# Gate segments, numerators and magnitudes reordered in the first iterations of an xLSTM-plus-MoE kernel

## The chip, the cores and the metric

The kernel runs on one core of one Trainium2 chip. The metric is the device time of one execution in microseconds (us), lower is better. The engines named below are PE (TensorE), DVE (VectorE), ACT (ScalarE), POOL (GpSimd) and SP (SyncE, which here only issues DMAs).

## The reference

Three parts follow each other on the same 1536 tokens (2 batches of 768), 320 wide (8 heads of 40):

```python
# 1: matrix-memory recurrence, per batch and head, over t
m_new = max(f_gate + m, i_gate)
f_stab, i_stab = exp(f_gate + m - m_new), exp(i_gate - m_new)
C = f_stab * C + i_stab * outer(v, k);  n = f_stab * n + i_stab * k
y = sigmoid(o_gate) * (C @ q) / max(|n . q|, 1)
# 2: rational activation between two matmuls, d_ff 2048
h = x @ w_in;  P = a0 + a1 h + a2 h^2 + a3 h^3;  Q = 1 + |b0||h| + |b1| h^2
x = (P / (Q + 1e-6)) @ w_out
# 3: RMS norm, gated unit, d_ff 1536
xn = x / rms(x) * rms_g;  y = (silu(xn @ w_gate) * (xn @ w_val)) @ w_out
```

## The kernel before, in words

Each engine has its own instruction list, written out by hand; the engines meet only at semaphores, and an engine that waits holds everything behind it in its list. There is no scheduler: the order in the code is the order on the engine.

The recurrence is computed in chunks of L = 128 steps. There are NT = 12 iterations `it`; iteration `it` is chunk c = it // 2 of batch b = it % 2. Per iteration PE makes the causal mask (`causal`, L1477) and adds the log weights (`log_weights`, L1492) in PSUM; ACT takes their exponential E (`weights`, L826); PE forms `scores` (L1467); DVE weighs the values (`weigh`, L1169) and multiplies scores by E (`probs`, L1176); PE forms the numerators within the chunk (`intra`, L1518), the part from earlier chunks (`carry`, L1505) and the state update (`updates`, L1528). DVE copies or adds up the numerators (`combine`, L1194/L1197), computes the reciprocal denominator (`denominators`: magnitude L1218, maximum with 1 L1219, reciprocal L1225) and writes the state (`state`, L1208/L1210). POOL multiplies by the output gate (`gated`, L576) and by the reciprocal (`normalised`, L585 and L588), decays the state (`decay`, L519) and fills a column of ones in each loaded value tile (`ones`, L509), for which `weigh` waits (semaphore `v_ready`). For the two last iterations ACT computes the magnitude instead of DVE (`magnitude`, L891).

The gates are [16, 768] and are handled in three segments, SEG: steps 0 to 127 (chunk 0, iterations 0 and 1), 128 to 255 (chunk 1, iterations 2 and 3), and the other 512 (chunks 2 to 5, iterations 4 on). For each segment i there is a chain over the engines:

- DVE: running maximum m_run (`gate_maxima`, L1079, a scan), steps a_step = f + m_prev - m (`gate_steps`, L1088 and L1089), their cumulative sum cumA (`gate_sums`, L1094, a scan), chunk ends (L1127);
- POOL: i_g - m_run (`input_steps`, L483), then minus cumA (`input_sums`, L489);
- ACT rounds both into gA and gB (`gate_rows_a` L738, `gate_rows_b` L743; POOL's L494 for segment 1), DVE and POOL add the low parts (`low_of_a` L1108, `low_of_b` L501);
- ACT then spreads gA over the heads for one iteration at a time (`spread`, L751, eight instructions; on DVE `spread_whole`, L1138, for iterations 0, 1 and 5). `log_weights(it)` on PE waits for this spread and for both low parts of its segment.

`gate_columns` (L1448) and `gate_ends` (L1456) on PE and `columns` on ACT (L770, L772) turn the chunk ends into the factors by which `carry` and `decay` go. PE also runs matmuls on a tile of zeros (`warm_up`, L1433), whose results nobody reads.

SP's list holds the loads; a ring of four tiles for q, k and for k, v is refilled when PE has used one. From iteration 9 on, the matmuls of part 2 (`first`, `second`) and then part 3 are mixed in.

## Time and profile before

| | us |
|---|---|
| median of 3 runs | 462.76 (462.76, 462.76, 466.35) |
| profiled execution | 463.35 |
| its span, first to last instruction | 461.3 |

| engine | busy us | share of the span |
|---|---|---|
| PE | 453.7 | 98% |
| DVE | 325.1 | 70% |
| ACT | 289.3 | 63% |
| POOL | 253.0 | 55% |

A row of the timeline gives start, duration, engine, line, operation, output<-input, count, and in brackets how long the engine was idle before it. A duration includes time in which the instruction was issued but held back. The recurrence takes about the first 90 us; the part that the change touches lies in the first 35.

### The profile page before, as it was taken

What the parts mean: (1) busy time and instruction counts of PE and PEld (TensorE: products, weight loads), DVE (VectorE), ACT (ScalarE), POOL (GpSimd) and SP (SyncE); (2) the same over time, 40 slices, a digit from 0 to 9 for tenths busy, and PEclk for the clock granted to TensorE, in tenths of its full rate; (3) what the DMA queues carried; (4) which work ended last, traced back from release to release, by engine and by line L of the source; (5) the groups of instructions that cost most, each with busy time, mean ns of one, the idle gap of its engine ahead of it and who ended that gap; (6) DMA issues with size and microseconds to landing.
All of it is one profiled execution on the core that took longest, in us unless ns stands there. A gap on an engine that the chain in (4) does not pass through costs nothing.

```text
span 461.3 us, 7426 instructions
## 1 busy us (share of the span) xinstructions
PE 453.7 (98%) x2670; PEld 397.9 (86%) x2670; DVE 325.1 (70%) x465; ACT 289.3 (63%) x472; POOL 253.0 (55%) x274
## 2 busy tenths in 40 slices
PE   8999999989999999999999999999999999999997
PEld 4889998878999888998889888888888888888886
DVE  7998997999999999999998363474433544533333
ACT  7789887899999999999997658432122222111111
POOL 5559699879988978888899655972000000000000
PEclk9999999999999999999999999999999999999999
DMA  8999920230000000000005030000010000100001
GB/s 229 349 319 287 266 88 2 92 137 1 1 1 0 3 0 1 0 1 1 1 0 217 2 137 2 0 1 0 0 58 0 1 0 1 57 3 0 1 0 57
DMA packets 8371, 26.76 MB, mean 58 GB/s; under 512 B 1216, under 2 KB 3136, under 8 KB 7824
## 3 DMA queue, kind: packets, MB, share of 16 engines
q1 hardware_dynamic: 8336, 26.30, 18.0%
q8 instruction: 21, 0.34, 0.3%
q14 instruction: 14, 0.11, 0.1%
HBM read 24.33 MB, written 1.97 MB: 57 GB/s over the span
## 4 chain that ended last, share of the span: by engine, by line
PE 85%; DVE 4%; issue 1%; ACT 1%; POOL 1%; DVEq 0%; ACTq 0%; POOLq 0%
PE ps L1666 7%; PE ps L1667 7%; PE ps L1668 7%; PE ps L1596 6%; PE ps L1597 6%; PE ps L1598 6%; PE ps L1572 4%; PE ps L1614 4%; PE ps L1570 4%; PE ps L1571 4%; PE ps L1615 4%; PE ps L1616 4%; PE ps L1670 4%; PE ps L1671 3%; PE ps L1518 2%; PE ps L1573 2%
## 5 line engine op out<-in xcount | busy, mean ns | idle before, releaser
L1026 ACT ACTIVATE ab<-ps 128x512 f32<-128x512 f32 x36 | 21.6, 599 | 117.5 <-PE ps L1671 117.5
L1382 DVE TENSOR_TENSOR ab<-ps,ab 128x512 f32<-128x512 f32 x36 | 24.9, 691 | 84.3 <-ACT ab L1026 84.3
L596 POOL TENSOR_TENSOR qq<-qq,ab 128x512 f32<-128x512 f32 x48 | 61.3, 1297 | 16.9 <-ACT qq L850 16.9
L602 POOL TENSOR_TENSOR g_lo<-cc,g_hi 128x512 fp32r<-128x512 f32 x48 | 61.9, 1309 | 5.0 <-ACT g_hi L874 4.8
L1596 PE MATMUL ps<-wo_hi,g_hi 128*128 128x320 f32 x192 | 59.8, 311 | 1.3 <-DVE cc L1249 1.0
L1597 PE MATMUL ps<-wo_lo,g_hi 128*128 128x320 f32 x192 | 59.3, 309 | 0.0
L1598 PE MATMUL ps<-wo_hi,g_lo 128*128 128x320 f32 x192 | 59.3, 309 | 0.0
L1614 PE MATMUL ps<-wo_hi,g_hi 128*128 128x320 f32 x136 | 42.0, 309 | 0.2 <-ACT g_hi L1034 0.2
L1616 PE MATMUL ps<-wo_hi,g_lo 128*128 128x320 f32 x136 | 42.0, 309 | 0.0
L1615 PE MATMUL ps<-wo_lo,g_hi 128*128 128x320 f32 x136 | 42.0, 309 | 0.0
L1596 PEld LDWEIGHTS ps<-wo_hi,g_hi 128*128 128x128 f32 x192 | 36.1, 188 | 4.6 <-ACT ab L833 1.3
L1244 DVE SCALAR_TENSOR_TENSOR cc<-cc,coef_a,ps 128x512 f32<-128x512 f32 x48 | 35.6, 743 | 5.0 <-ACT cc L842 5.0
L1570 PE MATMUL ps<-x_hi,w_hi 128*128 128x512 f32 x96 | 38.1, 397 | 0.3 <-DVE cc L1249 0.3
L1572 PE MATMUL ps<-x_hi,w_lo 128*128 128x512 f32 x96 | 38.1, 397 | 0.0
L1571 PE MATMUL ps<-x_lo,w_hi 128*128 128x512 f32 x96 | 37.9, 394 | 0.0
L1388 DVE TENSOR_TENSOR cc<-ps,ab 128x512 f32<-128x512 f32 x36 | 24.9, 691 | 18.1 <-PE ps L1671 17.9
L1597 PEld LDWEIGHTS ps<-wo_lo,g_hi 128*128 128x128 f32 x192 | 36.0, 188 | 1.7
L1249 DVE SCALAR_TENSOR_TENSOR cc<-cc,coef_a,ps 128x512 f32<-128x512 f32 x48 | 35.8, 747 | 1.4
L1598 PEld LDWEIGHTS ps<-wo_hi,g_lo 128*128 128x128 f32 x192 | 36.0, 188 | 0.0
L833 ACT ACTIVATE ab<-ps 128x512 f32<-128x512 f32 x48 | 28.5, 596 | 9.9 <-PE ps L1574 9.7
L1254 DVE SCALAR_TENSOR_TENSOR ab<-qq,one_eps,ps 128x1024 f32<-128x1024 f32 x24 | 30.7, 1278 | 4.7 <-ACT ps L866 4.4
L842 ACT ACTIVATE cc<-ps,coef_a 128x512 f32<-128x512 f32 x48 | 32.4, 678 | 0.0
(191 smaller groups left out, 1250.5 us busy)
## 6 DMA issues: line engine op xcount, KB each, us to landing
qk<-q_k_dram SPq DMA_DIRECT2D x12, 448.0 KB, 9.3
wo_raw<-w_out_dram SPq DMA_DIRECT2D x7, 640.0 KB, 8.4
kv<-kv_n_dram SPq DMA_DIRECT2D x10, 372.0 KB, 8.0
w_raw<-w_main_dram SPq DMA_DIRECT2D x4, 512.0 KB, 8.5
out_dram<-y_out SPq DMA_DIRECT2D x12, 160.0 KB, 1.8
sig_o<-o_n_dram SPq DMA_DIRECT2D x1, 1600.0 KB, 8.5
w2c_raw<-w_main_dram SPq DMA_DIRECT2D x1, 1536.0 KB, 6.3
rest_raw<-w_rest_dram SPq DMA_DIRECT2D x2, 512.0 KB, 9.0
```

The lines of the kernel that those rows point to most:

```text
L596: pool.tensor_tensor(qq[m % 2][:, h, :], qq[m % 2][:, h, :], ab[m % 2][:, h, :], ALU.mult)\
L602: pool.tensor_tensor(glo(n), cc[n // 2 % CR][:, n % 2, :], ghi(n).bitcast(F32), ALU.subtract)\
L1249: dve.scalar_tensor_tensor(part, part, coef_a[:, 1:2], hp[n], ALU.add, ALU.mult).then_inc(p_h, 1)
L1570: pe.matmul(hp[n], hi, x_hi[:, j, k, :], start=(k == 0), stop=False)
L1571: pe.matmul(hp[n], hi, x_lo[:, j, k, :], start=False, stop=False)
L1572: pe.matmul(hp[n], lo, x_hi[:, j, k, :], start=False, stop=False)
L1596: pe.matmul(acc[t], hi, wo1_hi[:, f, :], start=(f == 0), stop=False)
L1597: pe.matmul(acc[t], hi, wo1_lo[:, f, :], start=False, stop=False)
L1598: mm = pe.matmul(acc[t], lo, wo1_hi[:, f, :], start=False, stop=(f == FT1 - 1))
L1614: pe.matmul(acc[t], hi, wo2_hi[:, f, :], start=(f == 0), stop=False)
L1615: pe.matmul(acc[t], hi, wo2_lo[:, f, :], start=False, stop=False)
L1616: mm = pe.matmul(acc[t], lo, wo2_hi[:, f, :], start=False, stop=(f == FT2 - 1))
```

## The change

On DVE, iteration 0's `weigh` and `probs` come before the steps and sums of gate segment 1. Segment 2's maxima move from ahead of iteration 0 to behind `combine(0)`; its two step instructions leave DVE and become `steps_of_rest` on POOL, where DVE's `gate_sums(2)` waits for them (new semaphore `steps_done`); `gate_sums(2)` and the chunk ends come behind `combine(1)`, and `low_of_a(2)` behind `state(1)`. The magnitudes of iterations 0 and 1 are computed on ACT (`ON_ACT`). There are three reciprocal tiles instead of two. POOL's first iterations are written out: `normalised(0)` comes after the whole of segment 2's work. PE issues fewer zeros (8 matmuls behind the first 9 before, 4 now), takes `gate_columns` and `gate_ends` later, and `log_weights(2)` and `(3)` one place later. ACT rounds segment 2's cumA in iteration 2, next to gB.

```diff
--- before.py
+++ after.py
@@ -41,6 +41,7 @@
 FIRST_O = 2
 EARLY = (7, 8, 9, 10, 11, 17, 18, 19, 20, 21, 22, 24)
 ON_DVE = 5
+ON_ACT = (0, 1, NT - 2, NT - 1)
 WARM = 9
 ORDER = (0, 2, 4, 6, 1, 3, 5, 7)
 LAG1, LAG2 = 7, 2
@@ -128,7 +129,7 @@
         hU = [at(f"hU{i}", [P, H, D1]) for i in range(3)]
         den = at("den", [P, H])
         mag = at("mag", [P, 2, H])
-        rden = [at(f"rden{i}", [P, H]) for i in range(2)]
+        rden = [at(f"rden{i}", [P, H]) for i in range(3)]
         yo = at("yo", [P, HD])
         yo3 = yo[:, :].rearrange("p (h d) -> p h d", d=D)
         y = [at(f"y{i}", [P, KT * P]) for i in range(3)]
@@ -282,6 +283,7 @@
         act_seq = sem("act_seq")
         rounded_consts = sem("rounded_consts")
         maxima_done = sem("maxima_done")
+        steps_done = sem("steps_done")
         sums_done = sem("sums_done")
         b_done = sem("b_done")
         a_hi = sem("a_hi")
@@ -482,6 +484,13 @@
                 pool.wait_ge(maxima_done, i + 1)
                 own(pool.tensor_tensor(i_g[:, part], i_g[:, part], m_run[:, part], ALU.subtract))
 
+            def steps_of_rest():
+
+                part = SEG[2]
+                pool.wait_ge(maxima_done, 3)
+                own(pool.tensor_tensor(a_step[:, part], f_g[:, part], m_run[:, part.start - 1:part.stop - 1], ALU.add))
+                pool.tensor_tensor(a_step[:, part], a_step[:, part], m_run[:, part], ALU.subtract).then_inc(steps_done, 1)
+
             def input_sums(i):
 
                 part = SEG[i]
@@ -583,7 +592,7 @@
                 if it >= 3:
                     pool.wait_ge(t_done, it - 2)
                 own(pool.tensor_tensor(y[it % 3][:, 0:HD].rearrange("p (h d) -> p h d", d=D), yo3,
-                                       rden[it % 2][:, :].unsqueeze(2).to_broadcast([P, H, D]), ALU.mult))
+                                       rden[it % 3][:, :].unsqueeze(2).to_broadcast([P, H, D]), ALU.mult))
 
                 pool.tensor_scalar(y[it % 3][:, HD:KT * P], y[it % 3][:, 2 * P:HD], 1.0, None, ALU.mult)\
                     .then_inc(y_done, 1)
@@ -636,20 +645,23 @@
             high_of_b1()
             low_of_b(1)
             ones(1)
-            for it in range(NT - 2):
-                if it == 2:
-                    low_of_b(2)
-                if it == 0:
-                    input_steps(2)
-                if it < 2:
-                    ones(it + 2)
-                if B <= it < NT - 3:
+            ones(2)
+            gated(0)
+            steps_of_rest()
+            ones(3)
+            input_steps(2)
+            input_sums(2)
+            low_of_b(2)
+            decay(2)
+            normalised(0)
+            gated(1)
+            normalised(1)
+            for it in range(2, NT - 2):
+                if B < it < NT - 3:
                     decay(it)
-                if it >= 1:
+                if it >= 3:
                     gated(it - 1)
                     normalised(it - 1)
-                if it == 1:
-                    input_sums(2)
                 if it >= 2:
                     ones(it + 2)
                     pool.wait_ge(v_ready, it + 3)
@@ -901,13 +913,14 @@
                 if it == 0:
                     gate_rows_a(1)
                 if it == 2:
+                    gate_rows_a(2)
                     gate_rows_b(2)
                 if it < NT - B and it + 2 != ON_DVE:
                     spread(it + 2)
                 if it == 0:
                     columns(0)
-                if it == 1:
-                    gate_rows_a(2)
+                if it < 2:
+                    magnitude(it)
                 if it == 2:
                     columns(1)
                 if it == 3:
@@ -1091,6 +1104,8 @@
             def gate_sums(i):
 
                 part = SEG[i]
+                if i == 2:
+                    dve.wait_ge(steps_done, 1)
                 dve.tensor_tensor_scan(cumA[:, part], reset[:, part], a_step[:, part], 0.0, ALU.mult, ALU.add)\
                     .then_inc(sums_done, 1)
 
@@ -1147,9 +1162,6 @@
             spread_whole(0)
             spread_whole(1)
             gate_maxima(1)
-            gate_steps(1)
-            gate_sums(1)
-            chunk_ends(0)
 
             def coefficients():
                 dve.wait_ge(params_in, 48)
@@ -1214,15 +1226,15 @@
 
                 dve.wait_ge(hu_done, it + 1)
                 n_q = hU[it % 3][:, :, D]
-                if it < NT - 2:
+                if it not in ON_ACT:
                     own(dve.scalar_tensor_tensor(den[:, :], n_q, -1.0, n_q, ALU.mult, ALU.max))
                     own(dve.tensor_scalar(den[:, :], den[:, :], 1.0, None, ALU.max))
                 else:
-                    dve.wait_ge(mag_done, it - NT + 3)
+                    dve.wait_ge(mag_done, ON_ACT.index(it) + 1)
                     own(dve.tensor_scalar(den[:, :], mag[:, it % 2, :], 1.0, None, ALU.max))
-                if it >= 2:
-                    dve.wait_ge(y_done, it - 1)
-                dve.reciprocal(rden[it % 2][:, :], den[:, :]).then_inc(rden_done, 1)
+                if it >= 3:
+                    dve.wait_ge(y_done, it - 2)
+                dve.reciprocal(rden[it % 3][:, :], den[:, :]).then_inc(rden_done, 1)
                 dve.wait_ge(rden_done, it + 1)
 
             def split_out1(p):
@@ -1285,8 +1297,10 @@
 
             weigh(0)
             probs(0)
+            gate_steps(1)
+            gate_sums(1)
+            chunk_ends(0)
             low_of_a(1)
-            gate_maxima(2)
             for it in range(NT - 3):
                 if it >= B:
                     carried(it)
@@ -1295,16 +1309,16 @@
                 probs(it + 1)
                 if it + 2 == ON_DVE:
                     spread_whole(ON_DVE)
+                combine(it)
                 if it == 0:
-                    gate_steps(2)
-                combine(it)
+                    gate_maxima(2)
+                if it == 1:
+                    gate_sums(2)
+                    chunk_ends(1)
+                denominators(it)
+                state(it)
                 if it == 1:
                     low_of_a(2)
-                denominators(it)
-                state(it)
-                if it == 0:
-                    gate_sums(2)
-                    chunk_ends(1)
                 if it >= 3:
                     lo_of_x(it - 3)
                 if it == 6:
@@ -1676,31 +1690,33 @@
             causal(1)
             warm_up(1)
             log_weights(0)
-            warm_up(1)
             scores(0)
             log_weights(1)
+            causal(2)
+            warm_up(3)
+            scores(1)
+            intra(0)
             gate_columns(0)
             gate_ends(0)
-            warm_up(2)
-            causal(2)
-            warm_up(2)
-            scores(1)
-            intra(0)
-            log_weights(2)
             updates(0)
             for it in range(1, NT - 3):
-                if it >= 2:
+                if it == 2:
+                    causal(3)
+                    carry(2)
+                    log_weights(3)
+                elif it >= 3:
                     causal(it + 1)
                     log_weights(it + 1)
                     carry(it)
-                if it == 2:
-                    warm_up(2, 7, KT * P)
-                    gate_columns(1)
-                    gate_ends(1)
                 scores(it + 1)
+                if it == 1:
+                    log_weights(2)
                 if it >= 3:
                     transposes(it - 3)
                 intra(it)
+                if it == 2:
+                    gate_columns(1)
+                    gate_ends(1)
                 updates(it)
             causal(NT - 2)
             log_weights(NT - 2)
```

Place 1: DVE, from segment 1's maxima to the end of iteration 0's numerators, before. `m_run`, `a_step` and `cumA` are gate tiles, `wv` the weighed values, `E` the weights, `hU` the numerators, `ends` the chunk ends.

```order
L1079 SCALAR_TENSOR_TENSOR m_run<-gif,m_run 16x128
L1088 TENSOR_TENSOR a_step<-gif,m_run 16x128 [waits maxima_done]
L1089 TENSOR_TENSOR a_step<-a_step,m_run 16x128 [waits dve_seq]
L1094 SCALAR_TENSOR_TENSOR cumA<-reset,a_step 16x128 [waits dve_seq]
L1127 TENSOR_TENSOR ends<-cumA,ident 16x16 [waits consts,sums_done]
L1169 TENSOR_TENSOR wv_71<-kv_69,E_75 128x328 [waits exp_done,v_ready]
L1176 TENSOR_TENSOR E_75<-ps,E_75 128x1024 [waits s_done,wv_done,exp_done]
L1108 TENSOR_TENSOR gA<-cumA,gA 16x128 [waits a_hi]
L1079 SCALAR_TENSOR_TENSOR m_run<-gif,m_run 16x512
L1169 TENSOR_TENSOR wv_72<-kv_70,E_78 128x328 [waits exp_done,v_ready,maxima_done]
```

The same place now:

```order
L1092 SCALAR_TENSOR_TENSOR m_run<-gif,m_run 16x128
L1181 TENSOR_TENSOR wv_71<-kv_69,E_75 128x328 [waits exp_done,v_ready,maxima_done]
L1188 TENSOR_TENSOR E_75<-ps,E_75 128x1024 [waits s_done,wv_done,exp_done]
L1101 TENSOR_TENSOR a_step<-gif,m_run 16x128
L1102 TENSOR_TENSOR a_step<-a_step,m_run 16x128 [waits dve_seq]
L1109 SCALAR_TENSOR_TENSOR cumA<-reset,a_step 16x128 [waits dve_seq]
L1142 TENSOR_TENSOR ends<-cumA,ident 16x16 [waits consts,sums_done]
L1123 TENSOR_TENSOR gA<-cumA,gA 16x128 [waits a_hi]
L1181 TENSOR_TENSOR wv_72<-kv_70,E_78 128x328 [waits exp_done,v_ready]
L1188 TENSOR_TENSOR E_78<-ps,E_78 128x1024 [waits s_done,wv_done,exp_done]
L1206 COPY hU_88<-ps 128x328 [waits intra_done]
L1092 SCALAR_TENSOR_TENSOR m_run<-gif,m_run 16x512
```

Iteration 0's two instructions (`wv_71`, `E_75`) passed four gate instructions, and the 512-step maxima went from before iteration 1's `wv_72` to behind iteration 0's `hU_88`.

Place 2: DVE, iteration 1 behind its numerators, now.

```order
L1206 COPY hU_89<-ps 128x328 [waits intra_done]
L1109 SCALAR_TENSOR_TENSOR cumA<-reset,a_step 16x512 [waits steps_done]
L1142 TENSOR_TENSOR ends<-cumA,ident 16x64 [waits consts,sums_done]
L1234 TENSOR_SCALAR den<-mag 128x8 [waits mag_done,hu_done]
L1237 RECIPROCAL rden_94<-den 128x8 [waits dve_seq]
L1220 COPY C<-ps 40x164 [waits upd_done,rden_done]
L1220 COPY C<-ps 40x164
L1123 TENSOR_TENSOR gA<-cumA,gA 16x512 [waits a_hi]
```

Before, the 512-step sums stood ahead of iteration 2's values, and `gA<-cumA,gA` of 16x512 directly behind `hU_89`; both now come after it, with the state between them.

Place 3: POOL, from iteration 1's ones to the first output rows, before.

```order
L509 MEMSET kv_70 128x8 [waits kv_in1,low_b_done]
L483 TENSOR_TENSOR gif<-gif,m_run 16x512 [waits maxima_done]
L509 MEMSET kv_74 128x8 [waits kv_in2,pool_seq]
L509 MEMSET kv_77 128x8 [waits kv_in3]
L576 TENSOR_TENSOR yo<-hU_88,sig_o 128x320 [waits sig_done,hu_done]
L585 TENSOR_TENSOR y_96<-yo,rden_93 128x320 [waits rden_done,yo_done]
L588 TENSOR_SCALAR y_96<-y_96 128x64 [waits pool_seq]
L489 TENSOR_TENSOR gif<-gif,cumA 16x512 [waits sums_done,y_done]
L501 TENSOR_TENSOR gB<-gif,gB 16x512 [waits b_hi,b_done]
```

The same place now:

```order
L518 MEMSET kv_70 128x8 [waits kv_in1,low_b_done]
L518 MEMSET kv_74 128x8 [waits kv_in2]
L585 TENSOR_TENSOR yo<-hU_88,sig_o 128x320 [waits sig_done,hu_done]
L491 TENSOR_TENSOR a_step<-gif,m_run 16x512 [waits maxima_done,yo_done]
L492 TENSOR_TENSOR a_step<-a_step,m_run 16x512 [waits pool_seq]
L518 MEMSET kv_77 128x8 [waits kv_in3]
L485 TENSOR_TENSOR gif<-gif,m_run 16x512 [waits maxima_done]
L498 TENSOR_TENSOR gif<-gif,cumA 16x512 [waits sums_done,pool_seq]
L510 TENSOR_TENSOR gB<-gif,gB 16x512 [waits b_hi,b_done]
```

Two 512-step instructions were added, all four of segment 2 stand in one row behind iteration 0's `yo`, and iteration 0's output rows (`y_96`) went behind them.

## Rows read from the trace of the kernel before

**Rows 1.** The page: busy time by engine, granted PE clock in 40 slices.

```profile
PE 453.7 (98%) x2670; PEld 397.9 (86%) x2670; DVE 325.1 (70%) x465; ACT 289.3 (63%) x472; POOL 253.0 (55%) x274
...
PEclk9999999999999999999999999999999999999999
```

**Rows 2.** Timeline of PE: start us, duration us, line, output<-input, count, idle before.

```profile
1.17 4.02 PE L1433 MATMUL ps<-warm 128*128 128x512 bf16 x9 [1.17 <-DVE warm L1068]
...
12.32 1.16 PE L1467 MATMUL ps<-qk 40*128 40x128 f32 x16
...
23.07 1.16 PE L1467 MATMUL ps<-qk 40*128 40x128 f32 x16
...
27.38 0.63 PE L1492 MATMUL ps<-sel,gB 128*128 128x512 f32 x2
...
33.53 0.73 PE L1492 MATMUL ps<-sel,gB 128*128 128x512 f32 x2
...
45.38 0.62 PE L1492 MATMUL ps<-sel,gB 128*128 128x512 f32 x2
...
51.31 0.62 PE L1492 MATMUL ps<-sel,gB 128*128 128x512 f32 x2
```

**Rows 3.** Timeline of DVE, same columns.

```profile
9.83 0.41 DVE L1094 TENSOR_TENSOR_SCAN cumA<-reset,a_step 16x128 f32<-16x128 f32 x1
...
10.37 0.49 DVE L1169 TENSOR_TENSOR wv<-kv,E 128x328 f32<-128x328 f32 x1
10.95 1.23 DVE L1176 TENSOR_TENSOR E<-ps,E 128x1024 f32<-128x1024 f32 x1
...
12.52 1.27 DVE L1079 TENSOR_TENSOR_SCAN m_run<-gif,m_run 16x512 f32<-16x512 f32 x1
...
14.41 1.23 DVE L1176 TENSOR_TENSOR E<-ps,E 128x1024 f32<-128x1024 f32 x1
...
16.98 0.50 DVE L1194 COPY hU<-ps 128x328 f32<-128x328 f32 x1
...
19.36 1.21 DVE L1094 TENSOR_TENSOR_SCAN cumA<-reset,a_step 16x512 f32<-16x512 f32 x1
...
22.98 0.68 DVE L1108 TENSOR_TENSOR gA<-cumA,gA 16x512 fp32r<-16x512 f32 x1
23.69 1.12 DVE L1218 SCALAR_TENSOR_TENSOR den<-hU 128x8 f32<-128x8 f32 x1
24.85 0.17 DVE L1219 TENSOR_SCALAR den<-den 128x8 f32<-128x8 f32 x1
...
25.30 0.67 DVE L1208 COPY C<-ps 40x164 f32<-40x164 f32 x2
```

**Rows 4.** Timeline of POOL, same columns.

```profile
12.37 0.11 POOL L509 MEMSET kv<- 128x8 f32 x1
...
19.58 1.17 POOL L588 TENSOR_SCALAR y<-y 128x64 f32<-128x64 f32 x1
...
23.32 1.46 POOL L501 TENSOR_TENSOR gB<-gif,gB 16x512 fp32r<-16x512 f32 x1 [0.95 <-ACT gB L743]
...
25.58 0.80 POOL L576 TENSOR_TENSOR yo<-hU,sig_o 128x320 f32<-128x320 f32 x1
...
35.11 0.37 POOL L588 TENSOR_SCALAR y<-y 128x64 f32<-128x64 f32 x1
...
35.74 1.28 POOL L525 TENSOR_TENSOR w_lo<-w_raw,w_hi 128x512 fp32r<-128x512 f32 x1
```

**Rows 5.** Timeline of ACT, same columns.

```profile
8.20 1.02 ACT L826 ACTIVATE E<-ps 128x1024 f32<-128x1024 f32 x1 [0.46 <-PE ps L1492]
...
22.57 0.61 ACT L743 ACTIVATE gB<-gif 16x512 fp32r<-16x512 f32 x1
23.70 2.44 ACT L751 ACTIVATE sel<-gA,sel 64x128 fp32r<-64x128 f32 x8 [0.52 <-DVE gA L1108]
```

**Rows 6.** Timeline of PE at its longest idle stretch after the start.

```profile
95.97 0.39 PE L1596 MATMUL ps<-wo_hi,g_hi 128*128 128x320 f32 x1 [1.00 <-DVE cc L1249]
```

## The prediction, made before the changed kernel was run

> **What bounds the kernel now.** The page comes first: PE is busy 98% of the span at full granted clock, DVE 70% [rows 1]. So PE's list sets the end, and an edit counts by how far it moves PE's later instructions. PE's timeline then shows where it is bound by its own work: the log weights of iterations 7 and 8 follow each other in 5.93 us [rows 2], and from there on all hangs on PE and on what PE feeds. The early stretch is different. Scores(1) start at 12.32, right after DVE's probs(0), which end at 12.18 [rows 2, 3]; scores(3) start at 23.07 and follow probs(2). From the log weights of iteration 4, at 27.38, PE runs on alone except for one wait: the log weights of iteration 5 come 6.15 us later instead of about 5.9, about 0.3 us more [rows 2]. So what the change is worth is read in one number: **when do the log weights of iteration 4 start?** They need segment 2's gates: DVE's low_of_a(2), which ends at 23.66, then ACT's spread of 2.44 us, which ends at 26.14, 1.2 us before PE comes [rows 3, 5]. That 1.2 us is the slack of the gate chain, and the change makes this chain later by more than that.
>
> **What DVE and POOL do to each other.** The rows of DVE and POOL must be read together. The maximum with 1 and the magnitude work on the same 128x8, yet one took 0.17 and the other 1.12 us: the latter ended at 24.81, just after POOL's 23.32 to 24.78 [rows 3, 4]. POOL's copy of 128x64 took 0.37 alone and 1.17 when it began during DVE's 512-step sums; it ended 0.18 after them [rows 3, 4]. So a small or an all-SBUF DVE instruction and a POOL one hold each other up for a whole instruction, with about 0.15 us of their own time already done while they are held. Numerators, probs and state writes, which read PSUM, show full speed beside POOL. Whether POOL can hold one of DVE's scans no row shows: that DVE's scan holds POOL, one does. The Trainium skill (SBUF — State Buffer, "Who interferes with whom") says that a VectorE instruction with two SBUF inputs and a GpSimd one that reads SBUF exclude each other for the whole instruction, first come first served, and names no scans; extended to them it gives the sum below, not extended the second rival. The change puts four 512-element instructions of POOL in one row, where DVE has its own, so I take the mutual hold for all of them.
>
> **The sum, as a chain of times.**
> 1. *Iteration 0 ahead of segment 1's steps.* weigh(0) needs ACT's exponential, which ends at 9.22 [rows 5]; with 0.49 and 1.23 us [rows 3] and the handoffs, probs(0) end near 11.0 instead of 12.18. PE's scores(1) come 1.1 us earlier.
> 2. *Segment 1 later.* 1.81 us of work (10.37 to 12.18) passed it, so its sums end near 12.05 instead of 10.24 [rows 3]. Behind them POOL has input_sums, two parts of gB and then the ones of iteration 1, which began at 12.37, 2.13 us after the sums [rows 3, 4]; some 0.4 of it was a hold by weigh(0) that is gone now. So the ones are there near 13.8, and **weigh(1) waits for them**: a new wait, with probs(1) behind it. 13.8 + 0.49 + 1.23 and handoffs is 15.55, against 15.64 before (14.41 + 1.23). The 1.1 us are spent.
> 3. *Numerators ahead of segment 2.* combine(0), 0.50 us, is done at 16.05 instead of 17.48. The maxima of segment 2, 1.27 us, end at 17.3 instead of 13.79: 3.5 us later [rows 3].
> 4. *Steps on POOL.* POOL's gated(0), 0.80 us, is held by the maxima and ends near 17.95. Two instructions of 512 elements at 1.28 us, the nearest row (128 lanes instead of 16) [rows 4], with 0.07 between them: 20.65. DVE meanwhile gets probs(2) done near 20.85 and combine(1) near 21.35; that is the real gain of the edit: scores(3) could start near 21.6 instead of 23.07, and PE would be 1.5 us ahead.
> 5. *Sums of segment 2.* POOL goes on at once with ones(3) and input_steps(2), 20.95 to 22.25. DVE's sums come to it at 21.35 and are held: end 22.25 + 1.21 - 0.15 = 23.3, instead of 20.57 [rows 3].
> 6. *Denominator and state.* POOL's input_sums(2) then runs from 23.45 to 24.7; DVE's 128x8 maximum with 1 comes just behind and is held to 24.7; reciprocal 0.2 and state 0.67 make 25.65. The magnitude moved to ACT costs 0.2 us there, hidden behind spread(2) and (3), and saves DVE one instruction.
> 7. *Low parts.* ACT's gB, 0.61 us, is done at 25.35 and POOL's low_of_b(2) takes 25.45 to 26.75. DVE's low_of_a(2) stands behind the state now and comes at 25.65: held, it ends at 26.75 + 0.68 - 0.15 = 27.3; had it come first, 26.35. Before: 23.66.
> 8. *Spread and log weights.* Plus 2.44 us [rows 5] and handoffs: 29.9 or 28.95 instead of 27.38, so **+2.5 or +1.55 us**. PE, ready at 27.0, would wait there 2 to 3 us.
> 9. *Refund.* Iteration 5's wait of 0.3 us disappears (its spread on DVE is done before PE comes): +2.2 or +1.25. The two orders in step 7 hang on 0.2 us, which I can't decide; I take the middle, +1.75.
>
> The rest costs nothing: four zeros fewer give time only to a PE that waits anyway; the third reciprocal tile removes a wait that no row shows; normalised(0), last on POOL, is needed only by the transposes in iteration 3; the loads come up to 1.5 us earlier, and nobody waits for them; everything after the log weights of iteration 4 has the order of before and moves with it. The profiled execution took 463.35 us, 0.59 more than the median of the runs: 463.35 + 1.75 = 465.1, and on the scale of the median **464.5 us**.
>
> **Rivals.**
> - *Scans are not held.* Then step 5 ends near 22.5 and the rest follows 1.4 us earlier: +0.4 to +0.6, 463.3. For it: no row with a held scan. Against it: one that holds POOL.
> - *A gain.* DVE and POOL hardly meet, by luck of order. The sums end at 22.55, ACT's gA, behind iteration 3's exponential, near 23.7, low_of_a(2) at 24.35, the spread at 26.8, the log weights at 26.9: -0.5, with the refund -0.8, 462.0. More is not to be had, since ACT's list allows no earlier gA. Against it: two holds at this very place already before [rows 3, 4].
> - *The clock falls; this is the one that ends clearly slower.* The first nine matmuls of zeros took 4.02 us, near 0.43 each, the pace of the 1.2 GHz level, after an engine that had done nothing; later ones run at the 2.4 GHz level. The change takes away four zeros and adds waits of 0.5 to 0.9 us before scores(1) and (2) and the one of 2 to 3 us of step 8. It decides if that wait is long enough for the granted clock to drop. If a stretch like the first (4.3 us until 5.47) runs at half pace, 2.15 us are lost; if one iteration of 5.87 us does, 5.87. With +1.75: 466.7 to 470.4. Against it: an idle stretch of 1.00 us at 95 left the granted clock at full [rows 1, 6]; none is longer, so 2 to 3 us are untried. The Trainium skill (TensorE: Matmul & The Clock Gate, Part 1) says that the low level is the default and idleness brings it back; by it this rival is possible at step 8, and the kernel would lose the first stretch's price.
>
> **Chances and range.** The forecast has 0.55, scans not held 0.20, a gain 0.13, the clock 0.10; 0.02 stay for what I don't see. One per cent, 4.6 us, is what a measurement of this kernel tells from no change (one of its runs lies 3.6 us above the other two). Only the upper part of the clock's rival passes it: slower 0.08. No case reaches -1%: faster 0.02. The range runs from the gain, 461.9, to the low end of the clock's rival, 467.0; the forecast alone spans 463.9 to 465.3.
>
> **What will show it.** In the changed profile: DVE idle about 1.1 us before weigh(1), ended by POOL's ones (step 2); POOL's gated(0) far over 0.80 us long (4); DVE's 512-step sums longer than 1.21 us and ending past 22.5 (5); low_of_a(2) ending after 26 (7); PE idle over 1 us before the log weights of iteration 4, ended by ACT's spread (8); granted clock 1.00 in 24 to 36 us. The forecast is wrong if low_of_a(2) ends before 24.5: then PE doesn't wait and the kernel is faster. It is wrong too if the log weights of iterations 7 and 8 shift by another amount than those of iteration 4 less 0.3.

## The result

| | before | changed |
|---|---|---|
| median, us | 463.6 (6 runs) | 472.77 (6 runs, 471.63 to 484.06) |
| ratio of the runs | | 1.0204 [1.0165, 1.0243] |
| profiled execution, us | 463.35 | 471.82 |
| its span, us | 461.3 | 470.0 |
| mean granted clock | 0.999 | 0.978 |

The changed kernel is about 2% slower. The forecast was 464.5, the range ended at 467.0: wrong. Executions of one kernel differ by how long their granted clock was low, and ratios and their intervals leave out those over 1.5% above a kernel's fastest.

**The profile after.** Its page first: the busy times of DVE, ACT and POOL are those of [rows 1] within 1 us; PE is busy 8.3 us more with four matmuls less, and the granted clock, all nines in [rows 1], dips in two of the first slices.

```profile
PE 462.0 (98%) x2666; PEld 406.2 (86%) x2666; DVE 325.7 (69%) x461; ACT 289.8 (62%) x474; POOL 254.0 (54%) x276
...
PEclk9659999999999999999999999999999999999999
```

Windows of 2 us locate it. Columns: stretch, length, busy us (and instructions) of PE, PE's weight loads, DVE, ACT and POOL, granted clock, DMA share, GB/s.

```profile
10.00:12.00 2.00, 1.67 (x16) 0.89 (x16) 1.93 (x4) 0.97 (x1) 0.00 (x0) 1.00 1.02 281
12.00:14.00 2.00, 2.00 (x24) 1.88 (x20) 0.69 (x3) 1.37 (x5) 1.46 (x4) 1.00 1.04 266
14.00:16.00 2.00, 1.67 (x15) 1.44 (x14) 1.81 (x3) 1.65 (x7) 0.18 (x2) 1.00 1.03 343
16.00:18.00 2.00, 1.94 (x17) 1.74 (x18) 1.97 (x3) 0.22 (x1) 1.60 (x1) 0.60 1.03 305
18.00:20.00 2.00, 2.00 (x9) 1.81 (x9) 0.99 (x4) 0.93 (x1) 1.84 (x3) 0.50 1.12 357
...
36.00:38.00 2.00, 2.00 (x13) 1.67 (x14) 0.16 (x2) 0.87 (x1) 0.00 (x0) 0.78 0.77 214
38.00:40.00 2.00, 2.00 (x26) 1.88 (x26) 1.91 (x3) 1.97 (x3) 0.74 (x1) 1.00 1.01 343
```

The clock fell near 16.4 us to 0.50, the 1.2 GHz level, and was full again near 36.9: some 20 us. Before the fall PE lacks 0.33 us of work in each of two windows. In the kernel before it lacks less, and none in the second:

```profile
10.00:12.00 2.00, 1.85 (x10) 0.99 (x9) 1.88 (x4) 1.21 (x2) 1.44 (x3) 1.00 1.03 258
14.00:16.00 2.00, 2.00 (x18) 1.89 (x18) 1.91 (x3) 1.25 (x7) 1.57 (x2) 1.00 1.01 300
```

The timeline of PE, changed, shows where:

```profile
11.36 1.16 PE L1481 MATMUL ps<-qk 40*128 40x128 f32 x16 [0.33 <-DVE E L1188]
...
16.06 1.82 PE L1481 MATMUL ps<-qk 40*128 40x128 f32 x16 [0.40 <-DVE E L1188]
...
27.17 2.08 PE L1481 MATMUL ps<-qk 40*128 40x128 f32 x16
...
36.12 0.97 PE L1506 MATMUL ps<-sel,gB 128*128 128x512 f32 x2
...
60.09 0.63 PE L1506 MATMUL ps<-sel,gB 128*128 128x512 f32 x2
```

Scores(1) and (2) wait 0.33 and 0.40 us for DVE's probs. Then the scores of an iteration take 2.08 instead of 1.16 us. From scores(2) to the log weights of iteration 4 lie 20.06 us (16.06 to 36.12), before 10.81 (16.57, the row below, to 27.38, [rows 2]); the log weights of iteration 8 are 8.78 late (60.09 against 51.31), and the span ends 8.7 later. All of the loss lies in these 20 us.

```profile
16.57 1.16 PE L1467 MATMUL ps<-qk 40*128 40x128 f32 x16
```

The early steps of the forecast are there, in DVE's timeline:

```profile
9.99 1.22 DVE L1188 TENSOR_TENSOR E<-ps,E 128x1024 f32<-128x1024 f32 x1
...
14.10 0.50 DVE L1181 TENSOR_TENSOR wv<-kv,E 128x328 f32<-128x328 f32 x1 [1.20 <-POOL kv L518]
...
16.24 1.26 DVE L1092 TENSOR_TENSOR_SCAN m_run<-gif,m_run 16x512 f32<-16x512 f32 x1
...
28.84 0.68 DVE L1123 TENSOR_TENSOR gA<-cumA,gA 16x512 fp32r<-16x512 f32 x1 [2.48 <-ACT gA L750]
```

and in POOL's:

```profile
16.40 1.70 POOL L585 TENSOR_TENSOR yo<-hU,sig_o 128x320 f32<-128x320 f32 x1 [2.21 <-DVE hU L1206]
...
19.51 1.27 POOL L492 TENSOR_TENSOR a_step<-a_step,m_run 16x512 f32<-16x512 f32 x1
```

But the gate chain, on which the forecast rests, costs nothing here. ACT's spread for iteration 4 ends at 32.00, 4.1 us before PE, at half pace, gets to it:

```profile
29.56 2.44 ACT L763 ACTIVATE sel<-gA,sel 64x128 fp32r<-64x128 f32 x8 [0.23 <-DVE gA L1123]
```

### The profile page after: what moved, and what is told of

It is laid out like the page before. It is cut to its first block, busy times and chain, and to the rows that moved or that the text cites. A ratio compares the mean times of both kernels' runs of the same rounds, so it can differ in the third digit from the quotient of the medians.

```text
span 470.0 us, 7418 instructions
## 1 busy us (share of the span) xinstructions
PE 462.0 (98%) x2666; PEld 406.2 (86%) x2666; DVE 325.7 (69%) x461; ACT 289.8 (62%) x474; POOL 254.0 (54%) x276
## 3 DMA queue, kind: packets, MB, share of 16 engines
q1 hardware_dynamic: 8336, 26.30, 17.3%
## 4 chain that ended last, share of the span: by engine, by line
PE 90%; DVE 4%; POOL 2%; ACT 2%; issue 1%; POOLq 0%; DVEq 0%; ACTq 0%
PE ps L1680 7%; PE ps L1681 7%; PE ps L1682 7%; PE ps L1610 6%; PE ps L1612 6%; PE ps L1611 6%; PE ps L1532 4%; PE ps L1586 4%; PE ps L1628 4%; PE ps L1584 4%; PE ps L1585 4%; PE ps L1629 4%; PE ps L1630 4%; PE ps L1684 3%; PE ps L1685 3%; PE ps L1481 2%
## 5 line engine op out<-in xcount | busy, mean ns | idle before, releaser
L1039 ACT ACTIVATE ab<-ps 128x512 f32<-128x512 f32 x36 | 21.6, 599 | 117.5 <-PE ps L1685 117.4
```

## The experiments

A run **kept the clock** when its mean granted clock is 0.999 or more. The kernel before kept it in 36 of 95 runs (median of these 463.3, all runs 465.1, 462.7 to 477.5), and 11 of the 95 took over 468 us. The ratio leaves out the very runs that lost most to the clock (e2's rests on two of six), so it is to be read with the last column.

| run | kept the clock | median of these | median of all | ratio | over 468 us |
|---|---|---|---|---|---|
| changed kernel | 0 of 6 | | 472.8 | 1.0204 [1.0165, 1.0243] | 6 of 6 |
| e1 | 0 of 5 | | 473.9 | 1.0196 [1.0168, 1.0225] | 5 of 5 |
| e2 | 0 of 6 | | 471.9 | 1.0019 [0.9981, 1.0058] | 4 of 6 |
| e3 | 0 of 4 | | 471.8 | 1.0161 [1.0135, 1.0187] | 4 of 4 |
| e4 | 0 of 6 | | 471.9 | 1.0148 [1.0120, 1.0176] | 6 of 6 |
| e5 | 8 of 11 | 465.6 | 465.8 | 1.0036 [1.0009, 1.0063] | 2 of 11 |
| e6 | 6 of 11 | 464.9 | 465.9 | 1.0038 [1.0004, 1.0071] | 2 of 11 |
| e7 | 0 of 5 | | 474.9 | 1.0190 [1.0143, 1.0236] | 5 of 5 |
| e8 | 4 of 11 | 465.5 | 477.0 | 1.0032 [1.0004, 1.0060] | 6 of 11 |
| e9 | 0 of 6 | | 475.2 | 1.0192 [1.0140, 1.0243] | 6 of 6 |
| e10 | 1 of 12 | 465.0 | 472.4 | 1.0070 [1.0035, 1.0105] | 10 of 12 |
| e11 | 0 of 5 | | 471.7 | 1.0141 [1.0117, 1.0165] | 5 of 5 |
| e12 | 8 of 12 | 464.4 | 464.4 | 0.9991 [0.9976, 1.0006] | 3 of 12 |
| e13 | 8 of 11 | 463.2 | 463.3 | 0.9968 [0.9950, 0.9986] | 1 of 11 |
| e14 | 4 of 11 | 463.1 | 464.5 | 0.9979 [0.9958, 1.0001] | 4 of 11 |
| e15 | 5 of 11 | 464.1 | 464.7 | 0.9997 [0.9977, 1.0016] | 0 of 11 |
| e16 | 5 of 11 | 463.7 | 465.3 | 1.0002 [0.9980, 1.0024] | 1 of 11 |

### e1: zeros where PE waits for probs

```diff
             log_weights(0)
+            warm_up(1)
             scores(0)
...
-            warm_up(3)
+            warm_up(5)
             scores(1)
...
             updates(0)
+            warm_up(3, 6)
```

> The changed kernel with more zeros on PE: one matmul behind log_weights(0), five instead of three ahead of scores(1), three new ones (into bank 6) behind updates(0), where PE idled 0.4 us before 16.06. Nothing else differs. Theory A (the missing zeros and the short waits of PE before 16.06 made the clock fall at about 16.5 us, and the fall cost about 7 us): granted clock stays 1.00 in 16 to 28 us, log weights of iteration 4 start near 29 to 30 us instead of 36.12, time 464 to 466 us, that is before's plus the 1 to 2 us of the gate chain. Rival B (the clock fell because of the new order itself, not the zeros): clock 0.5 from about 16.5 us again, 471 to 473 us. Rival C (the zeros hold the clock at first, but the wait of 2 us or more ahead of the log weights of iteration 4 drops it there): full clock until about 28 us, half for some us behind, 467 to 471 us.

The clock stayed full at 16 us and up to 26.6, and so the forecast's chain can be read at full clock. PE, then DVE:

```profile
27.15 1.20 PE L1491 MATMUL ps<-mask,identr 128*128 128x512 f32 x2
29.98 1.22 PE L1506 MATMUL ps<-sel,gB 128*128 128x512 f32 x2 [1.63 <-ACT sel L763]
```

```profile
21.57 1.86 DVE L1109 TENSOR_TENSOR_SCAN cumA<-reset,a_step 16x512 f32<-16x512 f32 x1
...
23.61 1.26 DVE L1234 TENSOR_SCALAR den<-mag 128x8 f32<-128x8 f32 x1
...
25.84 1.61 DVE L1123 TENSOR_TENSOR gA<-cumA,gA 16x512 fp32r<-16x512 f32 x1
```

The sums are held (1.86 instead of the 1.21 of [rows 3]) and end at 23.43, behind a POOL instruction that ends at 22.35:

```profile
21.08 1.27 POOL L485 TENSOR_TENSOR gif<-gif,m_run 16x512 f32<-16x512 f32 x1
```

low_of_a(2) ends at 27.45, the log weights of iteration 4 start at 29.98: forecast 23.3, 27.3 and 29.9. But the clock fell near 26.6, 1.7 us before PE's wait there and with no idle time of PE in its rows since 7.4 us. Theory A held up to that point only, its time (464 to 466) did not come, and rival C's wait was not what dropped the clock in this run:

```profile
24.00:26.00 2.00, 2.00 (x21) 1.95 (x20) 1.89 (x5) 0.83 (x2) 1.20 (x2) 1.00 1.03 275
26.00:28.00 2.00, 2.00 (x12) 1.56 (x11) 1.97 (x3) 0.52 (x2) 1.92 (x2) 0.65 1.03 381
28.00:30.00 2.00, 0.37 (x2) 0.02 (x1) 1.91 (x3) 1.97 (x8) 1.83 (x4) 0.50 1.04 293
```

### e5 and e11: zeros at the second place, and without those in the wait

e5 adds to e1 (e11: the first of these two alone):

```diff
                 if it == 2:
+                    warm_up(3, 7, KT * P)
                     gate_columns(1)
...
                     causal(it + 1)
+                    if it == 3:
+                        zeros_behind_mask(6)
                     log_weights(it + 1)
```

> The changed order with the zeros of the first experiment (1 behind log_weights(0), 5 ahead of scores(1), 3 behind updates(0)), and besides 3 zeros ahead of gate_columns(1) and 6 added into the mask's banks between causal(4) and log_weights(4), where PE waited 1.63 us. If the falling clock is all that lies between the forecast (+1.75) and the result, the granted clock now stays at 1.00 from 6 us on, the log weights of iteration 4 start near 30.0, as in the first experiment, and those of iteration 7 near 47.7 (before: 45.38), so the time is 2.2 us above the kernel before's profiled 463.35: 465 to 466. If the zeros do not keep the clock there, it falls near 26 again and the time is 471 to 474. If the order costs by something else than these two, the log weights of iterations 4 and 7 are apart by more than 18.0 us at full clock.

> As e5 without the 6 zeros in the wait ahead of the log weights of iteration 4: there PE has nothing to do for about 1.6 us again, with 3 zeros ahead of gate_columns(1) still there. The time at full clock is that of e5, 465.6. If that wait itself drops the clock, as the third rival had it, the granted clock falls behind 28 us and the time is 469 to 474. If the thinner stretch 24 to 27 us dropped it in the first experiment, the clock now holds and the time is 465.6.

In e5's profiled run the clock is full throughout and the time 465.6, as expected, though PE still waits. Windows, then PE:

```profile
26.00:28.00 2.00, 2.00 (x19) 1.55 (x18) 1.97 (x3) 0.47 (x2) 1.92 (x2) 1.00 1.00 264
28.00:30.00 2.00, 1.46 (x7) 0.49 (x6) 1.91 (x4) 1.98 (x7) 1.83 (x4) 1.00 1.05 386
```

```profile
27.99 1.47 PE L1455 MATMUL ps<-warm 128*128 128x512 bf16 x6
...
30.03 0.73 PE L1510 MATMUL ps<-sel,gB 128*128 128x512 f32 x2 [0.58 <-ACT sel L763]
...
47.91 0.63 PE L1510 MATMUL ps<-sel,gB 128*128 128x512 f32 x2
```

The span is 463.8, against 461.3: **2.5 us is the price of the new order with these zeros at full clock**, nearly all of it the gate chain (iteration 4's log weights 2.65 later, iteration 7's 2.53). The early zeros have a small part in it: e8, with three fewer of them, has its log weights of iteration 4 at 29.81 instead of 30.03. So 6.2 of the 8.7 us come with the clock. e11 never kept the clock (four of its runs took 470.9 to 472.6, 5 to 7 us over e5, and one 480.8): all that it lacks against e5 is the six zeros in the wait, so these six zeros matter. That the clock falls in the unfilled wait, as the prediction's third rival had it, is argued and not shown: e11's profiled run fell already near 14.9 us, with the early zeros in place and no idle time of PE in its rows from 7.4 us to there.

```profile
14.00:16.00 2.00, 2.00 (x15) 1.92 (x15) 1.83 (x3) 1.61 (x7) 0.16 (x2) 0.73 1.02 310
```

### e7 and e6: the gate chain made early, with few zeros and with many

Maxima of segment 2 ahead of iteration 1, sums behind state(0), low_of_a(2) behind combine(1), gA in iteration 1, POOL's `ones(1)` ahead of `input_sums(1)` and its steps ahead of `gated(0)`. DVE's part:

```diff
             low_of_a(1)
+            gate_maxima(2)
...
                 combine(it)
-                if it == 0:
-                    gate_maxima(2)
                 if it == 1:
-                    gate_sums(2)
-                    chunk_ends(1)
+                    low_of_a(2)
                 denominators(it)
                 state(it)
-                if it == 1:
-                    low_of_a(2)
+                if it == 0:
+                    gate_sums(2)
+                    chunk_ends(1)
```

> The changed kernel, its few zeros kept, with the chain of segment 2 made early as in e6. If the clock falls because of the short waits ahead of scores(1) and (2) with few zeros, it falls near 16 again (granted clock 0.50 for 10 to 20 us) and the time is 468 to 472, though the gate chain is no later than before. If the late gate chain made the clock fall, it stays at 1.00 and the time is 462 to 464.

> As e5, but segment 2's chain is made early again: its maxima ahead of iteration 1's values (where DVE waited 1.2 us for POOL's ones), POOL's ones of iteration 1 ahead of its 128-step sums and its two steps ahead of yo, the 512-step sums behind state(0), ACT's gA in iteration 1, low_of_a(2) behind the numerators of iteration 1. The steps stay on POOL. If the lateness of this chain is what costs at full clock, low_of_a(2) ends near 23.5 instead of 27.5, PE does not wait for the log weights of iteration 4, and they start at 27.3 to 28.5 with PE's added zeros (9 x 0.22 us = 2.0 us of them now in PE's way), so 463.5 to 465.5. If POOL's steps by themselves cost (holds of weigh(1) for a whole 1.27 us), scores(2) start 1 us later than 16.46 and the time is near 466.

e7, on the changed kernel as it is, lost the clock near 15.3 us, between two waits ahead of scores like those of the changed kernel. The second one began at 15.85, after the fall, so only the first can have had a part in it:

```profile
10.00:12.00 2.00, 1.66 (x17) 0.92 (x17) 1.93 (x4) 0.93 (x1) 0.11 (x1) 1.00 1.03 247
...
14.00:16.00 2.00, 1.85 (x15) 1.56 (x14) 1.87 (x4) 1.53 (x7) 1.65 (x3) 0.82 1.03 254
16.00:18.00 2.00, 1.82 (x16) 1.81 (x16) 1.57 (x5) 0.22 (x1) 1.92 (x3) 0.50 1.04 356
```

```profile
11.32 1.16 PE L1481 MATMUL ps<-qk 40*128 40x128 f32 x16 [0.34 <-DVE E L1189]
...
16.18 2.08 PE L1481 MATMUL ps<-qk 40*128 40x128 f32 x16 [0.33 <-DVE E L1189]
```

So the late gate chain isn't what drops it, and curing the chain alone gains nothing: 474.9. With e5's zeros (e6) low_of_a(2) ends at 23.49, and PE no longer waits but has 9 zeros in its way: 464.9. e7 and e6 differ in zeros alone: all five runs of e7 took over 472 us, nine of eleven of e6 under 468. In e6's profiled run the clock fell all the same, near 26.7 us, and no idle time of PE stands in the rows ahead of it:

```profile
24.00:26.00 2.00, 2.00 (x18) 1.67 (x17) 1.87 (x5) 1.98 (x6) 0.89 (x1) 1.00 1.04 290
26.00:28.00 2.00, 2.00 (x16) 1.89 (x15) 1.93 (x4) 1.98 (x8) 1.92 (x3) 0.68 1.05 365
28.00:30.00 2.00, 2.00 (x7) 0.91 (x6) 1.07 (x4) 0.32 (x1) 1.75 (x4) 0.50 1.01 278
```

### e12: e6 with fewer zeros at the second place

```diff
-                    warm_up(3, 7, KT * P)
+                    warm_up(2, 7, KT * P)
...
-                        zeros_behind_mask(6)
+                        zeros_behind_mask(0)
```

> As e6 (segment 2's chain early, steps on POOL) with 2 instead of 3 zeros ahead of gate_columns(1) and none behind causal(4). At full clock the 7 zeros less are worth 7 x 0.22 us = 1.5 us of PE's time: 462.9 to 463.4 against e6's 464.7, level with the kernel before. If the clock falls near 26 again, as in e6's profiled run, 465 to 470.

464.4, with 8 runs within 0.15 us, and level with the kernel before on average (0.9991), having kept the clock in 8 of 12 runs against 7 of the 23 taken beside it; at full clock it is 1.1 us behind (spans of 462.4 against 461.3). Seven zeros less brought 0.5 of the 1.5 us expected. Its profiled run (474.4) lost the clock near 15.5 us, again with the early zeros in place and no idle time of PE from 7.4 us to there.

### e8: which of the early zeros

e5 without the three zeros more ahead of scores(0) and (1); only the 3 behind updates(0) stay.

> As e5, but ahead of 16 us only the 3 zeros behind updates(0) are added; the 3 that are missing against e5 (1 behind log_weights(0), 2 ahead of scores(1)) stay out. If the wait of 0.4 us ahead of scores(2) decides the fall at 16.4, the clock stays full and the time is that of e5, near 465.5. If it is the thinner stretch 8 to 12 us as a whole, the clock falls near 16 as in the changed kernel, and the time is 469 to 473.

4 of 11 kept the clock (465.5, as e5), with the wait of 0.33 us at 11 us as before and the one ahead of scores(2) filled; 7 didn't (467.5 to 478.2). Filling the second wait is enough in some runs, filling both in most (e5, 8 of 11). That both waits count is what this suggests; eleven runs of each don't prove it, and neither expectation held whole.

### e2, e13, e14: the zeros taken from the old order

e13 takes out the early ones, e14 the pair ahead of `gate_columns(1)`, e2 both:

```diff
             log_weights(0)
-            warm_up(1)
             scores(0)
...
             gate_ends(0)
-            warm_up(2)
             causal(2)
-            warm_up(2)
+            warm_up(3)
             scores(1)
...
-                    warm_up(2, 7, KT * P)
                     gate_columns(1)
```

The first three edits make 2 fewer zeros ahead of scores(1), not 4 as the expectation for e13 says.

> The kernel before with the zeros of the changed one: four fewer between 8 and 23 us (none behind log_weights(0), none between gate_ends(0) and causal(2), three instead of two ahead of scores(1), none ahead of gate_columns(1)); order on all engines as before. If zeros alone decide the clock (A in its plain form), it falls here too, near 16 us, and the time is 468 to 472 us. If the clock fell because zeros were missing and PE waited more at scores(1) and scores(2) as well (A with the new order's waits), the clock holds here and the time is 462.5 to 463.5 us; the removed zeros ahead of scores(3) give up to 0.4 us.

> The kernel before with only its early zeros cut to those of the changed kernel (4 fewer zeros ahead of scores(1), so 4 instead of 8 in all with the pair ahead of gate_columns(1) kept, which makes 6). No wait of PE is longer than 0.4 us. If the early zeros hold the clock near 26, or near 16, this kernel loses full-clock runs against the kernel before and its typical time is 466 to 476. If the late pair alone did it in the second experiment, the time is that of the kernel before: 463.1 in the full-clock runs, 465 in the middle.

> The kernel before without the 2 zeros ahead of gate_columns(1), early zeros kept. PE's later work comes up to 0.37 us earlier, so 462.7 in a full-clock run. If the late pair is what held the clock near 26, few runs are at full clock and the time is 466 to 472.

e13 kept the clock in 8 of 11 runs, the kernel before in 11 of the 34 beside it. So its middle is lower, **463.25 against 465.12**, 0.9968 [0.9950, 0.9986]; at full clock the two are level (463.2 and 463.3). PE's idle time in 10 to 14 us grew, but in 14 to 16 it has none:

```profile
10.00:12.00 2.00, 1.75 (x8) 0.90 (x8) 1.88 (x4) 1.12 (x2) 1.49 (x3) 1.00 1.04 322
12.00:14.00 2.00, 1.85 (x23) 1.64 (x22) 1.90 (x4) 1.53 (x6) 0.56 (x3) 1.00 1.01 277
14.00:16.00 2.00, 2.00 (x18) 1.89 (x18) 1.91 (x3) 1.27 (x7) 1.56 (x3) 1.00 1.05 420
```

e2 never kept it, and four of its six runs took 471.3 to 475.7 us: **with exactly the zeros of the changed kernel the old order loses most of its runs too**, and its median is 471.9 against the changed kernel's 472.8. In its profiled run (466.3) the clock was low from 26.4 to 29.9 us, not near 16, right behind a wait of 0.30 us:

```profile
26.06 1.32 PE L1528 MATMUL ps<-wv,kv 128*104 128x82 f32 x8 [0.30 <-DVE C L1208]
```

So its expectation has the time right (468 to 472) and the place, in this run, wrong. e14 has a like wait (0.28 us at 26.08) and its profiled run kept the clock; over its eleven runs it lies between, four of them over 470 and the middle at 464.5, under the 466 to 472 of its expectation. So the two zeros taken out early are harmless by themselves in the old order; those taken out late are not, most of all with the others gone. Where e2's longer runs fell isn't known.

### e15 and e16: more zeros in the old order

`warm_up(4, 7, KT * P)` for `warm_up(2, 7, KT * P)`; and `warm_up(2, 6)` behind `updates(0)`.

> The kernel before with 4 instead of 2 zeros ahead of gate_columns(1): 2 x 0.2 us in PE's way, 463.5 at full clock. If the kernel before's own spread (463.1 to 466.6) is the clock falling for a few us near 26, this one has more runs near 463.5 and its middle is below the kernel before's 465.0. If its spread has another cause, its middle is 465.4.

> The kernel before with 2 zeros more, behind updates(0): 0.43 us in PE's way, 463.5 at full clock. If a thin stretch near 16 us decides how the kernel before fares, its middle is below 465.0; if the stretch near 26 does, its middle is 465.4 as without them.

Neither differs from the kernel before (0.9997, 1.0002). e15 had no run over 465.3, where the kernel before has 4 of the 34 beside it over 468 (too few to tell the two apart), and its middle is 464.7: the spread of the kernel before near 465 isn't explained by this. e16's profiled run (470.9) had a low clock from 25.8 to 42.8 us with no idle time of PE in its rows from 16 us to there, so a busier stretch near 16 us doesn't protect the later one.

### e3, e4, e9, e10: other orders

e3 is e1 with segment 2's steps back on DVE behind state(0); e4 is e1 with POOL's `ones(1)` ahead of `input_sums(1)`; e9 and e10 have steps on DVE, `ones(1)` early, the sums behind state(0) and low_of_a(2) behind combine(1), and differ in zeros.

> As the first kernel of this call (more zeros), but the two 512-step instructions of segment 2 are back on DVE, behind state(0). With a full clock DVE does them in 1.35 us near 19 to 20.3 us, POOL is free for input_steps(2) from 18 us, and DVE's 512-step sums no longer meet a POOL instruction. If the four POOL instructions in one row, held against DVE's, make segment 2 late, low_of_a(2) ends 1 to 2 us earlier than with the steps on POOL, and the time is 0.8 to 1.5 us less. If PE's log weights of iteration 4 are bound by something else, the two are the same within 0.3 us.

> As the first kernel of this call (more zeros), but POOL fills the ones of iteration 1 ahead of input_sums(1) instead of behind low_of_b(1). If weigh(1) is held by these ones (DVE idle 1.20 us before 14.10 in the changed kernel), it starts near 13.0, everything on DVE behind it up to the 512-step maxima comes 1.0 us earlier, and with it the segment 2 chain: log weights of iteration 4 about 1 us earlier, time 0.7 to 1.1 us less than the first kernel. Rival: the gate chain is bound by POOL alone, which has gained nothing; less than 0.3 us.

> The changed order with its late gate chain taken out: segment 2's maxima and steps both on DVE behind combine(0), its sums behind state(0), ACT's gA in iteration 1, low_of_a(2) behind combine(1), POOL's ones of iteration 1 ahead of its 128-step sums. Zeros: 1 more behind log_weights(0), 5 instead of 3 ahead of scores(1), none behind updates(0), 2 ahead of gate_columns(1). weigh(1) then starts near 12.9 instead of 14.1, scores(2) near 15.9 instead of 16.5, and the log weights of iteration 4 near 26.7 if the clock holds (before: 27.38), so 462.3 to 463 against 463.1 of the kernel before's full-clock runs. If the missing zeros behind updates(0) let the clock fall, it falls between 15 and 27, and the time is 466 to 474.

> As e9 but with 4 zeros ahead of scores(1), 2 behind updates(0), 2 ahead of gate_columns(1) and 2 behind causal(4). If the clock holds in both, this one is slower than e9 by the 4 zeros that stand in PE's way, 3 x 0.22 us or 0.7 us: 463 to 463.7. If the zeros behind updates(0) are what holds it, as e8 showed for the changed order, this one has full-clock runs and e9 has none.

All but one run of e10 lost the clock. In the profiled runs e3 lost it at 26.5 us and e4 at 30.9, 1.5 us behind its wait of 1.80 us for the log weights of iteration 4 (at 29.40); e9 lost it at 20.8, right behind a wait of 1.13 us of updates(1) for the state. e3 missed its expectation: low_of_a(2) ends at 28.32, 0.87 later than in e1 and not earlier, since the steps on DVE hold up iteration 2. In e4 it ends at 26.86, 0.59 earlier, between expectation and rival. e9 and e10 were meant to beat the kernel before and don't: in e10's one run that kept the clock, DVE's 512-step maxima and two steps behind each other make the state late, so that updates(1) wait 0.83 us for it and scores(3) 0.42 for probs(2), and the log weights of iteration 4 come at 29.08.

## Why the prediction was wrong

- **Steps 1 to 8 held.** probs(0) ended at 11.21 (forecast 11.0), weigh(1) waited 1.20 us for POOL's ones (1.1), the maxima ended at 17.50 (17.3), POOL's steps at 20.78 (20.65), and in e1, whose clock was full to 26.6, the sums at 23.43, low_of_a(2) at 27.45 and the log weights at 29.98. One side remark of step 4 was too good: scores(3) start at 22.56 in e1, not near 21.6. The sum doesn't use it.
- **Step 9 was a little too kind:** the refund measured 0.15, not 0.3 us, and the two orders of step 7 came out the late way. At full clock the change costs 2.5 us with e5's zeros (median of the runs that kept the clock 465.6 against 463.3, so 2.3), the forecast took 1.75 and left 2.2 open.
- **The step that failed is "the rest costs nothing: four zeros fewer give time only to a PE that waits anyway".** PE's time they do not cost, the clock they do. With zeros put back and more added, and nothing else changed, 8 of 11 runs keep the clock at 465.6 (e5), where the changed kernel keeps it in 0 of 6 at 472.8; e6 against e7 shows the same with the gate chain early. And the four zeros taken from the old order, alone, give 471.9, with 0 of 6 keeping it (e2). The new order has its part too: e11, with at least as many zeros as the kernel before at every place and five more in all, kept it in 0 of 5. So either half of the change is enough to lose it in most runs.
- **What the waits do is less sure.** The waits ahead of scores(1) and (2), which the forecast expected (0.5 to 0.9 us) and did not price, are 0.33 and 0.40 us, and after the second the clock fell. A fall near 15 to 16 us came in both profiled runs with neither wait filled (changed kernel and e7; in e7 before the second wait). With zeros there, five profiled runs passed that place (e1, e3, e4, e5, e6) and two did not (e11 at 14.9, e12 at 15.5, both behind the first place, filled, and ahead of the second). So a wait is not needed for a fall there, and that the two waits raise its odds is likely but not shown apart from the zeros.
- **The rival had the right mechanism in the wrong place and at the wrong size.** It was put at step 8's wait and priced at 2.15 to 5.87 us on top of 1.75. Zeros at that place matter too (e11 against e5, 5 to 7 us), though no profiled run shows a fall inside the wait. Its price of 2.15 us rests on the pace of the first nine zeros; the granted clock reads 1.00 in those rows (windows 0 to 4 us), so the price was not read from a row at the low level. In the changed kernel the clock was gone some 12 us earlier and stayed low for some 20 us, which made 10.81 us of work last 20.06; and the gate chain then cost nothing, being ready 4.1 us before PE. The two terms didn't add here: the larger hid the other.
- **The argument for giving it 0.10 was the error of judgement:** one idle stretch of 1.00 us in dense work at 95 us had left the clock alone [rows 6]. The stretch up to 30 us is not the one at 95; what makes the difference no run shows. That the kernel before had a run 3.6 us over the others was in view as well; 59 of its 95 later runs lost some clock, so it stood near the edge, and a change that takes zeros from PE there should have had the larger chance.
- *Scans are not held* is refuted: 1.86 against 1.21 us (e1). *A gain* did not come at any zeros.

**What stays open:** what decides, in a given execution, whether the clock falls. e1, e6, e11, e12 and e16 lost it with no idle time of PE in the rows just before, e10's profiled run kept it through a wait of 0.83 us, and equal programs differ from run to run. Open too is how the loss divides between zeros and order: exactly the old zeros in the new order were never run.

## What to carry to other kernels

Matmuls of zeros in a stretch where the engine waits on others are not idle filler: before counting their removal as free, give the granted clock a term of its own, and test the removal alone in the old order first (e2's median is 6.8 us over that of the 95 runs of the kernel before, the changed kernel's 7.7). A clock that falls in an early stretch costs nearly the time of the work in it once more (1.86 times here, for 20 us); how long it stays low varied from 3.4 us (e2) to 27.3 us (e9), and nothing here says what ends it. Compare this cost with the other delays in the same stretch: here the later chain vanished behind it. And repeat the kernel before often enough to see how near the edge it stands: none of the new orders reached it at full clock (the nearest, e12, is 1.1 us behind), and the lowest middle, e13's (1.9 us under it), came with the old order and two zeros fewer.

## What the runs showed of the hardware

- In the changed kernel the granted clock fell after waits of 0.33 and 0.40 us and stayed at the 1.2 GHz level for 20 us in which PE shows no idle time (windows 18 to 36 us: 2.00 of 2.00 busy). The Trainium skill (TensorE: Matmul & The Clock Gate, Part 1) names long idle gaps as what brings the low level back, and tells besides of a kernel with short, frequent gaps whose clock went back and forth; the changed kernel's trace is nearer to the second, with no gap over 0.40 us between 8 us and the fall. The falls of e1, e6, e11, e12 and e16, with no gap recorded just before them, fit neither.
- At the low level PE's rows are 1.7 to 1.8 times as long, not twice: scores 2.08 us for 1.16, the mask 1.20 for 0.71; the whole stretch was 1.86 times as long (20.06 for 10.81, in nearly the same order; with exactly the same list and full clock e4 goes from scores(2) at 16.46 to the start of the last mask at 26.88, where the changed kernel goes from 16.06 to 35.12: 1.83 times).
- DVE's scan is held by a POOL instruction: 1.86 instead of 1.21 us, with POOL's 1.27 us of 16x512 from 21.08 ahead of it.
